# A gated recurrence and two feed-forward layers on one core: raw weights in four buffers, weight sums, down weights and input splits in other tiles, and the last group's remainders on VectorE

## The reference, cut to what matters

```
sig = 1.0 / (1.0 + np.exp(-f_logit))
f = lower_bound + (1.0 - lower_bound) * sig
for t in range(S):                       # S = 6080 tokens, D = 256
    h = f[:, t] * h + (1.0 - f[:, t]) * x[:, t]
    y[:, t] = h
h = y @ w_in0                            # 256 x 2048
z = (h * (1.0 / (1.0 + np.exp(-1.702 * h)))) @ w_out0      # 2048 x 256
h = z @ w_in1
g = np.where(h >= 1, h, np.where(h <= -1, 0, (h + 1) ** 2 / 4))
out = g @ w_out1
```

## Time and profile before

| | |
|---|---|
| median of 3 runs | 1034.95 us (1034.68 to 1036.28) |
| profiled execution: time, span | 1034.48 us, 1032.7 us |
| PE busy | 1010.4 us, 98% of the span, 4392 matmuls |
| DVE, ACT, POOL busy | 73%, 70%, 57% |
| DMA | 130.76 MB, mean 127 GB/s |
| mean granted TensorE clock | 0.996 of full speed |

### The profile page before, as it was taken

The page is one execution under the profiler, slowest core; times in us unless marked ns, Lnnn a source line. Parts: engine busy times, 40 slices in busy tenths (PEclk is TensorE's granted clock), DMA queues, the critical chain, the costliest instruction groups (busy, mean ns, idle before and its releaser), DMA issues.

```text
span 1032.7 us, 14219 instructions
## 1 busy us (share of the span) xinstructions
PE 1010.4 (98%) x4392; PEld 824.1 (80%) x4392; DVE 751.5 (73%) x1047; ACT 720.6 (70%) x1334; POOL 583.8 (57%) x475
## 2 busy tenths in 40 slices
PE   4999999999999999999999999999999999999998
PEld 4988888887888888888888888888888888888886
DVE  7877856785578897667888677789766456667666
ACT  6766777666677587676777777768766666777665
POOL 4657767756677456437646536646644754673433
PEclk9999999999999999999999999999999999999999
DMA  8655655415633232533232243222233323222421
GB/s 266 203 212 192 243 209 197 163 62 184 224 138 107 72 108 72 189 113 106 73 105 75 97 164 130 90 81 98 74 106 113 108 72 108 72 107 72 149 72 41
DMA packets 53180, 130.76 MB, mean 127 GB/s; under 512 B 6000, under 2 KB 16752, under 8 KB 52080
## 3 DMA queue, kind: packets, MB, share of 16 engines
q1 hardware_dynamic: 53104, 129.85, 36.0%
HBM read 106.82 MB, written 23.00 MB: 126 GB/s over the span
## 4 chain that ended last, share of the span: by engine, by line
PE 92%; DMA 2%; issue 2%; POOL 2%; DVE 1%; ACT 1%; POOLq 0%; SPq 0%; DVEq 0%; ACTq 0%
PE chain L505 24%; PE acc L546 16%; PE acc L547 16%; PE acc L543 16%; PE pair L505 12%; PE single L505 7%; DMA w_main<-blocks_kept 1%; POOL g_lo L1390 1%; DMA blocks_kept<-w_main 1%; DVE gate L1040 0%; DMA gate<-f_logit_dram 0%; POOL xin1lo L1364 0%; DVE state L1069 0%; ACT g_hi L826 0%; POOL w_main L1320 0%
## 5 line engine op out<-in xcount | busy, mean ns | idle before, releaser
L1390 POOL TENSOR_TENSOR g_lo<-g_act,g_hi 128x512 fp32r<-128x512 f32 (+1 forms) x271 | 367.2, 1356 | 407.1 <-ACT g_hi L826 403.6
L786 ACT ACTIVATE spare<-chain 128x512 f32<-128x512 f32 x240 | 143.2, 596 | 180.8 <-PE chain L505 180.0
L1156 DVE TENSOR_TENSOR spare<-pair,spare 128x512 f32<-128x512 f32 x160 | 109.9, 687 | 147.9 <-PE pair L505 147.3
L826 ACT ACTIVATE g_hi<-g_act 128x512 fp32r<-128x512 f32 (+1 forms) x271 | 169.3, 625 | 10.7 <-DVE g_act L1180 8.4
L505 PE MATMUL chain<-xin1hi,w_main 128*128 128x512 f32 x416 | 162.9, 396 | 0.6 <-DMA w_main<-blocks_kept 0.6
L546 PE MATMUL acc<-g_lo,w_down1hi 128*128 128x512 f32 (+1 forms) x384 | 150.6, 392 | 2.2 <-POOL g_lo L1390 2.2
L543 PE MATMUL acc<-g_hi,w_down0hi 128*128 128x512 f32 (+1 forms) x384 | 150.0, 391 | 1.4 <-ACT g_hi L826 1.4
L546 PE MATMUL acc<-g_lo,w_down0hi 128*128 128x512 f32 (+1 forms) x384 | 150.2, 391 | 0.2 <-DVE g_lo L1191 0.2
L547 PE MATMUL acc<-g_hi,w_down0lo 128*128 128x512 f32 (+1 forms) x384 | 150.3, 391 | 0.0
L547 PE MATMUL acc<-g_hi,w_down1lo 128*128 128x512 f32 (+1 forms) x384 | 150.3, 391 | 0.0
L543 PE MATMUL acc<-g_hi,w_down1hi 128*128 128x512 f32 (+1 forms) x384 | 150.2, 391 | 0.0
(11 more groups left out here) (117 smaller groups left out, 2039.4 us busy)
## 6 DMA issues: line engine op xcount, KB each, us to landing
w_main<-sums_kept SPq DMA_DIRECT2D x80, 512.0 KB, 3.7
w_main<-blocks_kept SPq DMA_DIRECT2D x80, 256.0 KB, 3.1
w_a<-blocks_kept SPq DMA_DIRECT2D x80, 128.0 KB, 3.9
zout<-w_in_dram SPq DMA_DIRECT2D x32, 256.0 KB, 3.5
blocks_kept<-w_main SPq DMA_DIRECT2D x16, 512.0 KB, 3.5
w_main<-blocks_kept SPq DMA_DIRECT2D x16, 512.0 KB, 4.3
sums_kept<-xin0hi SPq DMA_DIRECT2D x16, 512.0 KB, 2.9
out_dram<-zout SPq DMA_DIRECT2D x10, 512.0 KB, 5.2
```

The costliest lines, as they stand in the source:

```text
L786: act.activation(snap[k][:, 0:n], chain[g % 2][:, 0:n], ACT.Copy).then_inc(s_snap, 1)
L826: act.activation(g_hi[h % 4][:, 0:n], activated(h), ACT.Copy).then_inc(s_ghi, 1)
L1156: dve.tensor_tensor(to[:, 0:n], bank[:, 0:n], snap[(0, 2, 1)[k]][:, 0:n], ALU.add).then_inc(s_evac, 1)
L1390: pool.tensor_tensor(g_lo[h % 4][:, 0:n], g_act[h % 4][:, 0:n], g_hi[h % 4][:, 0:n].bitcast(F32), ALU.subtract).then_inc(s_glo_pool, 1)
```

## The change

Four edits, none of which alters the work of PE. (1) `raw_up` gets two more buffers in a new tile `raw_more`; four loads are issued ahead in stage 0 and in stage 1, and the wait in `load_raw_up` is for four groups back. (2) In stage 0 ACT's exp and bias steps of chunk 1 move: the first half ahead of `first_hi(3)` in the prologue, the second to s = 2 and 3; the down splits of groups 2 to 7 come two tiles later. (3) In stage 2 the down splits go to s = 1, 5, 9, 11, and the input splits and one `t_sum` move by one tile. In stage 4 the jobs move from s = 1, 5, 9, 13 to s = 1, 3, 5, with one job more in stage 3, and the first input splits come later. (4) `by_dve` gives DVE all four remainders of the last group.

```
 for _g in range(4):
     SUMS_AT[1, 4 * _g + 1] = _g
-    SUMS_AT[4, 4 * _g + 1] = NG + 2 + _g
-for _g in range(6):
+for _g in range(3):
+    SUMS_AT[4, 2 * _g + 1] = NG + 3 + _g
+for _g in range(7):
     SUMS_AT[3, _g] = 4 + _g
...
-    return h % 4 == C12 or h % 4 == C11 and is_plain(stage_of(h)) or h == TILES_BEFORE[NS] - 1
+    return h % 4 == C12 or h % 4 == C11 and is_plain(stage_of(h)) or h >= TILES_BEFORE[NS] - 4
...
-        raw_up = [zout[:, r * 512:(r + 1) * 512] for r in range(2)]
+        raw_more = sbuf("raw_more", [P, 2 * 512], F32)
+        raw_up = [(zout, raw_more)[r // 2][:, r % 2 * 512:(r % 2 + 1) * 512] for r in range(4)]
...
             def load_raw_up(l, g):
-                if (l, g) >= (0, 2):
-                    sp.wait_ge(s_blocks, made_n(l, g) - 2)
-                sp.dma_start(raw_up[g % 2], up_source[l][g]).then_inc(s_raw_up[g % 2], 16)
+                if (l, g) >= (0, 4):
+                    sp.wait_ge(s_blocks, made_n(l, g) - 4)
+                sp.dma_start(raw_up[g % 4], up_source[l][g]).then_inc(s_raw_up[g % 4], 16)
...
                 if si == 1:
...
-                    if g == 4:
-                        load_raw_up(1, 0)
-                        load_raw_up(1, 1)
+                    if g in (4, 5):
+                        load_raw_up(1, 2 * (g - 4))
+                        load_raw_up(1, 2 * (g - 4) + 1)
                 if si == 2:
                     keep_blocks(1, g)
-                    if g + 2 < NG:
-                        load_raw_up(1, g + 2)
-                    if g < 3:
-                        load_raw_down(1, g + 5)
+                    if g + 4 < NG:
+                        load_raw_up(1, g + 4)
+                    if g in (0, 1, 3):
+                        load_raw_down(1, (5, 6, 0, 7)[g])
```

In ACT's `plain_fill` for stage 0, and in its prologue:

```
-                    if s % 2 == 1 and s // 2 + 2 < NG:
-                        down_hi(0, s // 2 + 2)
-                    if s < 2:
-                        exp_step(1, s)
-                        inc_step(1, s)
+                    if s % 2 == 1 and 3 <= s < 15:
+                        down_hi(0, s // 2 + 1)
+                    if s == 2:
+                        exp_step(1, 1)
+                    if s == 3:
+                        inc_step(1, 1)
...
             first_hi(2)
+            exp_step(1, 0)
+            inc_step(1, 0)
             first_hi(3)
```

In POOL's `plain_fill`, and at the end of DVE's program:

```
                 if si == 4:
-                    if s in (6, 7):
-                        x_lo(5, (B11, B21)[s - 6])
-                    if s in (9, 10, 11, 12, 14):
-                        x_lo(5, {9: B22, 10: T1, 11: T3, 12: T2, 14: T4}[s])
+                    if 8 <= s <= 14:
+                        x_lo(5, (B11, B21, B22, T1, T3, T2, T4)[s - 8])
...
             g_step(end - 3)
+            lo_step(end - 4)
             g_step(end - 2)
+            lo_step(end - 3)
+            g_step(end - 1)
             lo_step(end - 2)
-            g_step(end - 1)
             lo_step(end - 1)
```

More of the change, by code:

```diff
@@ L238, in build @@
         s_tsum, s_zsum, s_xhi, s_xlo = sem("s_tsum"), sem("s_zsum"), sem("s_xhi"), sem("s_xlo")
-        s_raw_up, s_raw_down = [sem(f"s_raw_up{r}") for r in range(2)], [sem(f"s_raw_down{r}") for r in range(2)]
+        s_raw_up, s_raw_down = [sem(f"s_raw_up{r}") for r in range(4)], [sem(f"s_raw_down{r}") for r in range(2)]
         s_raw_sums = [sem(f"s_raw_sums{r}") for r in range(2)]
@@ L452, in _ @@
             sp.dma_start(state[:, 1024:2048], x[BASE[1]:BASE[2]].rearrange("(p m) -> p m", p=P)).then_inc(s_x_early[1], 16)
+            load_raw_up(0, 2)
+            load_raw_up(0, 3)
             for G in range(GROUPS):
@@ L456, in _ @@
                     keep_blocks(0, g)
+                    if g + 4 < NG:
+                        load_raw_up(0, g + 4)
                     if g + 2 < NG:
-                        load_raw_up(0, g + 2)
                         load_raw_down(0, g + 2)
@@ L751, in blocks_hi @@
             def blocks_hi(l, g):
-                act.wait_ge(s_raw_up[g % 2], 16 * (NG // 2 * l + g // 2 + 1))
+                act.wait_ge(s_raw_up[g % 4], 16 * (NG // 4 * l + g // 4 + 1))
                 if (l, g) >= (0, 2):
@@ L757, in blocks_hi @@
                         act.wait_ge(s_kept_blocks[g - 2], 16 * (l + 1))
-                act.activation(w_main[g % 2][:, 0:4, 0, :], raw_up[g % 2].rearrange("p (a f) -> p a f", a=4),
+                act.activation(w_main[g % 2][:, 0:4, 0, :], raw_up[g % 4].rearrange("p (a f) -> p a f", a=4),
                                ACT.Copy).then_inc(s_blocks_hi, 1)
@@ L874, in plain_fill @@
                         blocks_hi(1, s // 2 + 1)
-                    if s % 2 == 1 and s < 8:
-                        down_hi(1, 4 + s // 2)
+                    if s in (1, 5, 9, 11):
+                        down_hi(1, {1: 4, 5: 5, 9: 6, 11: 7}[s])
                     if s == 3:
@@ L882, in plain_fill @@
                         x_hi(3, (B11, B21)[s])
-                    if 7 <= s <= 11:
-                        x_hi(3, (B22, T1, T3, T2, T4)[s - 7])
+                    if s in (7, 8, 9, 10, 12):
+                        x_hi(3, {7: B22, 8: T1, 9: T3, 10: T2, 12: T4}[s])
                 if si == 4:
@@ L891, in plain_fill @@
                         f_step(3, 3)
-                    if s in (5, 6):
-                        x_hi(5, (B11, B21)[s - 5])
+                    if s in (6, 7):
+                        x_hi(5, (B11, B21)[s - 6])
                     if s in (8, 9, 10, 11, 13):
@@ L1199, in plain_fill @@
                         recurrence(2, (0, 1, 3, 5)[s - 12])
-                    if s % 2 == 1 and s // 2 + 2 < NG:
-                        down_lo(0, s // 2 + 2)
+                    if s % 2 == 1 and 3 <= s < 15:
+                        down_lo(0, s // 2 + 1)
                 if si == 1:
@@ L1210, in plain_fill @@
                         z_evac(1, 0)
[L1211 to L1214, removed]
+                    if s in (7, 8, 10):
+                        t_sum(3, {7: 0, 8: 1, 10: 2}[s])
+                    if s in (1, 5, 9, 11):
+                        down_lo(1, {1: 4, 5: 5, 9: 6, 11: 7}[s])
                 if si == 4:
@@ L1319, in blocks_lo @@
                 pool.wait_ge(s_blocks_hi, made_n(l, g))
-                pool.tensor_tensor(w_main[g % 2][:, 0:4, 1, :], raw_up[g % 2].rearrange("p (a f) -> p a f", a=4),
+                pool.tensor_tensor(w_main[g % 2][:, 0:4, 1, :], raw_up[g % 4].rearrange("p (a f) -> p a f", a=4),
                                    w_main[g % 2][:, 0:4, 0, :].bitcast(F32), ALU.subtract).then_inc(s_blocks, 1)
@@ L1412, in plain_fill @@
                         x_lo(3, (B11, B21)[s - 1])
-                    if 8 <= s <= 12:
-                        x_lo(3, (B22, T1, T3, T2, T4)[s - 8])
+                    if s in (8, 9, 10, 11, 13):
+                        x_lo(3, {8: B22, 9: T1, 10: T3, 11: T2, 13: T4}[s])
                 if si == 4:
-                    if s in (6, 7):
-                        x_lo(5, (B11, B21)[s - 6])
-                    if s in (9, 10, 11, 12, 14):
-                        x_lo(5, {9: B22, 10: T1, 11: T3, 12: T2, 14: T4}[s])
+                    if 8 <= s <= 14:
+                        x_lo(5, (B11, B21, B22, T1, T3, T2, T4)[s - 8])
                 if (si, s) in SUMS_AT:
```

## The result

The changed kernel takes 1029.59 us (median of 6 runs, 1028.28 to 1032.34) beside 1034.93 of the kernel before, measured with it: ratio 0.9949, 95% interval 0.9934 to 0.9964. A second measurement on another chip gave 0.994 (0.9928 to 0.9953), 1028.64 us. I had predicted 1030.7 with a range of 1026.8 to 1033.8. The profiled execution, the fastest of the six, took 1028.28 us, 6.20 less than that of before (1034.48); by the medians the gain is 5.3 and 6.2.

A forecast was written before the change was run, and what follows sets the result against it. TensorE was taken to bound the kernel, with about 9.5 us of waits and low clock within reach. Terms -2.4 - 1.35 + 0.3 - 0.8 = -4.25 us, from a median of 1034.95, gave 1030.7, range 1026.8 to 1033.8.

The forecast's parts named there:

- part 2: Stage 2: earlier raw loads and moved DVE work remove PE's two waits for POOL's remainders, -1.35 us.
- part 3: Stage 4: the 2.4 us weight wait goes, 2.7 us of new waits come, the clock falls again; net +0.3 us.
- Part 1: Start of stage 0: tile 0's remainder comes 0.9 us earlier and the clock stays up, 1.5 more; -2.4 us.
- from the clock: Start of stage 0: the TensorE clock no longer falls to half rate after the shorter wait, gaining 1.5 us.
- after 1.4 plus 0.23 it fell: Start of stage 0: the clock fell after these waits, stayed after 0.8, so a 0.95 us wait should keep it up.
- I count both waits: Stage 2: PE's wait of 0.8 us and the later one of about 0.5 both go, 1.35 us.
- My bound of 0.5: Stage 2: the smallest gain allowed for, 0.5 us, if DVE stays as late.
- the two new waits: Stage 4: PE waits 0.6 us for group 3's weights at s = 6 and 2.1 for group 4's at s = 8.
- The chain that I drew: Stage 4: `weight_sums` delays `sums_lo`, then store, raw load and weight load, so weights reach PE late, by 2.1 us for group 4.
- waits, but the clock stays: Stage 4: waits come as computed but the clock stays up after 2.1 us, 1029.2 us; no chance of its own given.
- Part 4: Last group: with POOL idle, DVE's `g_step` takes 0.68 us and PE's whole wait of 0.81 goes; -0.8 us.
- rival on the slower side: Stage 0: late down remainders hold up SP's queue, then ACT and PE, 1.5 us in each of six groups; 1039.7, chance 0.05.

The follow-up runs named there:

- buffers alone: The kernel before with only the four raw buffers and their load order on SP's queue; 1032.75 us against 1034.87, ratio 0.9986.
- tail alone: The kernel before with only the last group's four remainders on DVE; 1033.67 us against 1034.87, ratio 0.999.
- start undone: The changed kernel with stage 0's order (exponentials and increments of chunk 1, down splits) as in the kernel before; 1031.79 us against 1034.34, ratio 0.9977.
- splits at old tiles: The changed kernel with only stage 0's down splits (ACT's and DVE's) back at their old tiles; 1030.88 us against 1035.17, ratio 0.9959.
- inputs spread: The changed kernel with stage 2's last five input remainders on POOL at tiles 9, 11, 13, 14 and 15; 1027.78 us.
- the changed kernel again: The changed kernel, nothing altered, measured a second time on another chip; 1028.64 us, ratio 0.994.
- sums first: The changed kernel with POOL's remainder of the weight sums ahead of the next job's sums in the plain stages; 1027.41 us.
- both: The changed kernel with the edits of sums first and inputs spread together; 1026.26 us against 1034.34, ratio 0.9915.

## Why the prediction held, and where it did not

The sum was -4.25; the medians gained 5.3 and 6.2, the profiled executions 6.20. That the time lies in the range is in part luck: part 2 gave 1.1 us less than I had, part 3 2.4 more, and the two errors pull apart.

*Part 1, -2.4; stage 0 gave -2.30.* The size was right, the reason half. 0.67 us at tile 0 (I took 0.9) is there. The 1.5 "from the clock" is not shown. The step that failed is "after 1.4 plus 0.23 it fell": it fell so in two traces (before, buffers alone) and not in two others with a first wait of 1.32 and 1.44 (tail alone, start undone). And a fall did not lengthen the stage: 42.32 and 42.27 with it, 42.17 without. What makes about half of the gain is the down splits' later place, which I had costed at nothing beyond tile 0. At the old tiles ACT waits for the raw down weights at full clock (5.7, 3.4 and 4.4 us in tail alone, start undone and splits at old tiles, from 12 to 40 us; nothing in after), and PE is held up at 44 to 46 us, where it is not in after.

*Part 2, -1.35; stage 2 gave -0.21.* "I count both waits" failed. The first went, worth 1.10 with its surroundings. The second I put down to DVE's down remainders; it is POOL's crowding, and the new order added a wait of 0.61. My bound of 0.5 was still too hopeful.

*Part 3, +0.3; stage 4 gave -2.06.* The wrong sign: the two new waits and the clock were too dear in my sum. The chain that I drew is the true one. The stage begins 3.0 us earlier than in before, so my two loads were due at 232.8 and 240.4; they left at 232.56 and 240.09. But PE lost 0.25 and 1.5 us to them where I had 0.6 and 2.1 (in the other traces of this order up to 0.57 and 1.28 to 2.02). The clock stayed up, the rival "waits, but the clock stays". Some 0.95 us less of waiting and a fall of 1.3 to 1.6 (worked out below) make up the 2.4 by which the part was off. And the old order's cost I knew from one execution: without the fall it has a second wait, of 0.54 to 1.19 in four traces, so there it costs 2.3 to 3.4 us of waiting.

*Part 4, -0.8; measured -1.06 to -1.09.* Right in its mechanism; the bracket of the wait was too small a measure. The rule of the Trainium skill, Perfetto Trace Analysis, section "Optimizing Scalar/DVE Operations", that moving work between GpSimd and VectorE may not help, did not decide here: GpSimd was left with nothing to collide with. In stage 2, where both work, this case's trace agrees that the two hold each other up: the down remainder of VectorE at 125.63 us takes 1.61 us beside GpSimd's work, and one at 36.85, with GpSimd idle, 0.68. It is not VectorE that pays each time: the one at 120.79 takes 0.68, and GpSimd's remainder beside it 1.63, where the same step takes 1.15 at 106.23 in "inputs spread".

*Stage 1, nothing; it gave -0.59.* The weight wait there was 0.22 after 0.64, and varies by itself: the changed kernel again took 44.96, longer than before.

No rival on the slower side showed: PE's only waits in stage 0 of after are 0.52 us for an input remainder, which was 0.49 before, and the 0.76 at tile 0.

## What to carry to other kernels

Cut the timeline at the first matmul of each stage and compare lengths over several traces: that tells a lasting gain from a wait that only moves, which no list of waits does. Before a low clock is priced, ask what PE would reach earlier without it; here a transfer or a busy helper was next in line and took most of it back. When a helper is late, count all it has to do between two deadlines of PE: spreading five input remainders over more tiles removed two waits, one of which the change's own new order of that stage had made.

## What was not expected of the hardware

The clock's fall is not settled by the length of the wait. In stage 4 it fell behind waits of 2.40, 2.02 and 1.76 us, and not behind 2.53, 2.25, 2.16 and 1.75; behind 1.28 to 1.54 it stayed in five traces of five. What decides between is open.

What a fall costs the kernel can be less than its rows say. Of 62 executions of the kernel before, beside the experiments, 22 with a mean clock of 0.996 or 0.997 took 1035.5 us on average and 20 with 0.999 or 1.000 took 1034.0: 1.5 us for what counts up to two falls of 1.5 each. Of the changed kernel's first six executions the four at 1.000 took 1028.3 to 1030.3 us, the two at 0.998 took 1031.0 and 1032.3.

The stage itself pays in full. Stage 4 less the waits that its trace brackets took 46.2 to 46.3 us in nine traces at full clock (those of "sums first" and "both", with another order, left out), and 47.5, 47.8 and 47.8 in the three with a fall: 1.3 to 1.6 us. In the kernel before, a second wait of 0.54 to 1.19 us stands there at full clock and not behind the fall, so that a good part comes back; in the changed kernel's order of stage 4 no such wait was seen, and the two traces with a fall took 49.77 and 50.39 us (with waits some 0.5 and 1.1 us longer) where five without took 47.7 to 48.0.
